# Up projection of two mixture-of-experts layers split into 2x2x2 blocks, seven block products for eight

## The reference

```python
for t in range(S):                       # B, H, S, D = 2, 8, 768, 64
    state = gamma * state + einsum('bhd,bhe->bhde', k[:, :, t], v[:, :, t])
    y[:, :, t] = scale * einsum('bhd,bhde->bhe', q[:, :, t], state)
for e in range(E):                       # N, D, F = 1536, 512, 1024; E = 8, then 4
    h = np.maximum(x @ w1[e], 0.0)       # up projection
    out += P[:, e:e + 1] * (h @ w2[e])   # down projection
```

## Time and profile before

| | |
|---|---|
| median of three runs | 1670.83 us (1670.52 to 1671.59) |
| span of the profiled execution | 1668.0 us |
| TensorE busy | 1658.2 us (99%), 7656 matmul records |
| VectorE, ScalarE, GpSimd busy | 490.5, 296.9, 44.1 us |
| DMA | 64.23 MB, mean 39 GB/s |

### The profile page before, as it was taken

The page is one execution under the profiler, slowest core; times in us unless marked ns, Lnnn a source line. Parts: engine busy times, 40 slices in busy tenths (PEclk is TensorE's granted clock), DMA queues, the critical chain, the costliest instruction groups (busy, mean ns, idle before and its releaser), DMA issues.

```text
span 1668.0 us, 18690 instructions
## 1 busy us (share of the span) xinstructions
PE 1658.2 (99%) x7656; PEld 1374.9 (82%) x7656; DVE 490.5 (29%) x793; ACT 296.9 (18%) x487; POOL 44.1 (3%) x62
## 2 busy tenths in 40 slices
PE   8999999999999999999999999999999999999999
PEld 7988888888888888888888888888888888888887
DVE  5752332332232132132133123225123213213211
ACT  2321221221121121121121122113112112112111
POOL 3310000000000000000000000001000000000000
PEclk9999999999999999999999999999999999999999
DMA  8520110010011011011011011001001101101000
GB/s 177 122 102 1 51 51 0 3 67 32 0 50 50 0 50 50 0 50 50 0 50 50 0 50 51 0 0 66 36 0 51 50 0 50 50 0 50 25 25 25
DMA packets 62157, 64.23 MB, mean 39 GB/s; under 512 B 40240, under 2 KB 42416, under 8 KB 62128
## 3 DMA queue, kind: packets, MB, share of 16 engines
q1 hardware_dynamic: 47248, 58.99, 10.7%
q10 hardware_dynamic: 14880, 4.83, 1.2%
HBM read 60.67 MB, written 3.15 MB: 38 GB/s over the span
## 4 chain that ended last, share of the span: by engine, by line
PE 99%; issue 1%; DVE 0%; POOL 0%; SPq 0%; POOLq 0%; DVEq 0%
PE bank L707 16%; PE bank L705 16%; PE bank L682 16%; PE bank L686 16%; PE bank L684 16%; PE bank L709 16%; PE bank L580 2%; PE bank L607 1%; PE bank L592 1%; PE bank L598 1%; PE bank L569 0%; PE bank L659 0%; PE bank L563 0%; PE bank L642 0%; PE bank L644 0%
## 5 line engine op out<-in xcount | busy, mean ns | idle before, releaser
L707 PE MATMUL bank<-w_lo,h_hi 128*128 128x512 f32 x1152 | 453.7, 394 | 0.0
L705 PE MATMUL bank<-w_hi,h_hi 128*128 128x512 f32 x1152 | 452.3, 393 | 0.0
L682 PE MATMUL bank<-x_hi,w_hi 128*128 128x512 f32 x1152 | 448.5, 389 | 0.0
L684 PE MATMUL bank<-x_lo,w_hi 128*128 128x512 f32 x1152 | 448.2, 389 | 0.0
L686 PE MATMUL bank<-x_hi,w_lo 128*128 128x512 f32 x1152 | 448.1, 389 | 0.0
L709 PE MATMUL bank<-w_hi,h_lo 128*128 128x512 f32 x1152 | 447.2, 388 | 0.0
L358 ACT ACTIVATE h_hi<-bank 128x512 fp32r<-128x512 f32 x288 | 172.2, 598 | 1255.2 <-PE bank L686 1255.2
L505 DVE SCALAR_TENSOR_TENSOR h_lo<-bank,h_hi 128x512 fp32r<-128x512 f32 x288 | 199.2, 692 | 545.1 <-ACT h_hi L358 545.1
L515 DVE SCALAR_TENSOR_TENSOR acc<-bank,gate,acc 128x512 f32<-128x512 f32 x144 | 101.0, 750 | 566.0 <-PE bank L709 566.0
L705 PEld LDWEIGHTS bank<-w_hi,h_hi 128*128 128x128 f32 x1152 | 216.3, 188 | 50.0
L709 PEld LDWEIGHTS bank<-w_hi,h_lo 128*128 128x128 f32 x1152 | 216.2, 188 | 48.4
(11 more groups left out here) (62 smaller groups left out, 251.6 us busy)
## 6 DMA issues: line engine op xcount, KB each, us to landing
w_raw<-in_moe_w SPq DMA_DIRECT2D x23, 2048.0 KB, 8.1
k_in<-in_k SPq DMA_DIRECT2D x12, 256.0 KB, 3.8
q_in<-in_q SPq DMA_DIRECT2D x12, 256.0 KB, 4.5
v_in<-in_v ACTq DMA_DIRECT2D x10, 256.0 KB, 3.0
w_raw<-in_moe_w ACTq DMA_DIRECT2D x4, 512.0 KB, 4.8
out<-acc SPq DMA_DIRECT2D x2, 1024.0 KB, 4.3
out<-acc SPq DMA_DIRECT2D x4, 256.0 KB, 2.1
mask<-in_c_mask SPq DMA_DIRECT2D x1, 512.0 KB, 6.3
```

Of the source, the lines that this page charges most:

```text
L682: nc.tensor.matmul(up_bank[f % 2][:, :], w1_hi[:, c, fs], x_hi[:, c, cols], start=(c == 0), stop=False)
L684: nc.tensor.matmul(up_bank[f % 2][:, :], w1_hi[:, c, fs], x_lo[:, c, cols], start=False, stop=False)
L705: nc.tensor.matmul(down_bank[u][:, :], h_hi[:, f, rows], w2_hi[:, f, :], start=(f == 0), stop=False)
L707: nc.tensor.matmul(down_bank[u][:, :], h_hi[:, f, rows], w2_lo[:, f, :], start=False, stop=False)
```

## The change

Each half expert (512 of the 1024 columns of w1, and the matching rows of w2) is now a unit, 24 in all. Within it the up projection is seen as a 2x2 block matrix times a 2x2 block matrix: features in two halves of 256, hidden columns in two halves of 256, and tokens in two halves, which are the two batches. Instead of eight block products it makes seven, of sums and differences of blocks, and adds their results:

```diff
+PRODUCTS = [
+    (W_A11, X_B11, ON_X, True),
+    (W_S2, X_T2, ON_X, False),
+    (W_S3, X_T3, ON_Y, True),
+    (W_S1, X_T1, ON_X, False),
+    (W_S4, X_B22, ON_X, False),
+    (W_A12, X_B21, ON_Z, True),
+    (W_A22, X_T4, ON_Y, False),
+]
...
-        x_hi = sb("x_hi", [P, DC, NTOK], F32R)
...
-        w1_hi = sb("w1_hi", [P, DC, FF], F32R)
...
+        x_hi = sb("x_hi", [P, 7, 2, SEQ], F32R)
...
+        w1_hi = sb("w1_hi", [P, 7, 2, 2 * P], F32R)
...
+        w1_sum = sb("w1_sum", [P, 3, 2, 2 * P])
...
+            ups = sb("ups", [P, 2, 3, BLK], F32, moe)
```

TensorE goes twice through each unit, with blocks of 384 tokens of each batch (`PAIRS` = 2, `CPB` = 3). X, Y and Z are PSUM bank pairs, one bank for each half of 128 hidden columns:

```diff
+            def up(k, p, first=False, gates_out=False, x2=None):
...
+                for n, (w, x, kind, start) in enumerate(PRODUCTS):
+                    if p == 0:
+                        pe.wait_ge(w1_ready, 4 * k + {W_A11: 1, W_S1: 1, W_S2: 2, W_S3: 2, W_S4: 3}.get(w, 4))
...
+                    for half in range(2):
+                        if first and n == 0 and half == 0:
+                            pe.wait_ge(xlo_ready, 3 * CPB)
+                        if first and n == 5 and half == 0:
+                            pe.wait_ge(y_drained, STEPS)
+                        if n == 1:
+                            pe.wait_ge(copied, copies_before(k, p) + (half + 1))
+                        elif n == 3:
+                            pe.wait_ge(copied, copies_before(k, p) + (2 + half + 1))
+                        elif n == 4:
+                            pe.wait_ge(copied, copies_before(k, p) + (4 + half + 1))
+                        elif n == 6:
+                            pe.wait_ge(summed, sums_before(k, p) + (half + 1))
...
+                        for kc in range(2):
+                            nc.tensor.matmul(o, w1_hi[:, w, kc, fs], x_hi[:, x, kc, at],
+                                             start=start and kc == 0, stop=False, skip_group_check=True)
+                            nc.tensor.matmul(o, w1_hi[:, w, kc, fs], x_lo[:, x, kc, at],
+                                             start=False, stop=False, skip_group_check=True)
+                            last = nc.tensor.matmul(o, w1_lo[:, w, kc, fs], x_hi[:, x, kc, at],
+                                                    start=False, stop=kc == 1, skip_group_check=True)
+                        last.then_inc(up_done, 1)
```

ScalarE copies three partial results of X per half to SBUF (`hidden_copy`, behind products 0, 1 and 3) and still applies ReLU; VectorE adds Y or Z to them (`hidden_sum`, 6 per pass of 384 columns) and makes `h_lo` (8 per pass):

```diff
+            def hidden_copy(k, p, prod, half, slot):
+                act.wait_ge(up_done, ups_before(k, p) + (2 * prod + half + 1))
+                nc.scalar.copy(ups[:, half, slot, :], up_psum(ON_X, half)).then_inc(copied, 1)
...
+            def hidden_sum(k, p, n, half, slot, kind):
+                nc.vector.tensor_tensor(ups[:, half, slot, :], up_psum(kind, half), ups[:, half, slot, :],
+                                        ALU.add).then_inc(summed, 1)
```

VectorE makes the sums of the w1 blocks (`w1_sums`, four of 512 columns) and now also casts w2 (`split_w2`, four operations of 1024 columns). The loads of w1 and w2 are halves of 1 MB each, all from SP's queue. VectorE's order for one unit:

```diff
+            def unit(k, gate, col, how="add"):
+                split_w2(k)
+                hidden(k, 0)
+                down(k, 0, gate, col, how)
+                w1_sums(k + 1)
+                hidden(k, 1)
+                down(k, 1, gate, col, how, split_next=True)
```

The x blocks' sums (`x_sums`, four of 256 columns) and low parts (512, 512 and 768 columns) are GpSimd's, per chunk of 128 tokens of both batches, in the attention and between the layers (there the first two low parts are VectorE's). `y_dec` has three buffers in turn. In the attention the loops are written out; VectorE's queue towards its end:

```diff
+            for s in range(STEPS):
+                c, b = s // BATCH, s % BATCH
+                mask_scores(s)
...
+                y_out(s, b, c)
+                if s == STEPS - 4:
+                    w1_sums(0, first=True)
+                if s == STEPS - 2:
...
+                    split_w1_low(0, 0)
+                    split_w1_low(0, 1)
+            split_w1_low(0, 2)
+            split_w1_low(0, 3)
```

The start of the experts on TensorE and on ScalarE, where `y1_high` makes the high parts of the last five x blocks of a chunk (`logits` waits for all low parts of x, `xlo_ready` 3 * CH; TensorE's lines stand first):

```diff
+            up(0, 0, first=True)
+            logits()
...
+            pe.wait_ge(logits_out, 2)
+            down(0, 0, first=True)
+            gates()
+            up(0, 1, gates_out=True)
...
+            unit(0, 0)
+            y1_high(CH - 1)
+            logits_to_sbuf()
```

More of the change, by code:

```diff
@@ L187, in _ @@
             load_v(0, 1)
-            with sp.Fori(0, CH - 1) as c:
+            for c in range(CH - 1):
                 for b in range(BATCH):
@@ new lines, in scale_acc, with down @@
+            def scale_acc(p):
+                for u in range(2 * CPB):
+                    i = row_of(p, u)
+                    dve.wait_ge(acc_written, downs_before(1, p) + (u + 1))
+                    nc.vector.tensor_scalar(acc[:, i, :], acc[:, i, :], gate1[:, i, 0:1], None,
+                                            ALU.mult).then_inc(acc_scaled, 1)
+            def down(k, p, gate, col, how="add", split_next=False):
+                for u in range(2 * CPB):
+                    add_expert(k, p, u, gate, col, how)
+                    if split_next and u < 4:
+                        split_w1_low(k + 1, u)
@@ L557, in _ @@
+            down(L2_LAST, 1, gate2, E2 - 1)
         @block.tensor
@@ new lines, in down @@
+            def down(k, p, first=False, x2=None):
+                if p == 0:
+                    pe.wait_ge(w2_ready, 2 * k + 2)
+                for u in range(2 * CPB):
+                    b, rows = (1 if u < CPB else 0), slice(u % CPB * P, (u % CPB + 1) * P)
+                    if not (first and u < 2):
+                        pe.wait_ge(acc_written, downs_before(k, p) + (u - 1))
+                    for n, f in enumerate([2, 0, 3, 1] if b else [0, 1, 2, 3]):
+                        if u == 0 or u == CPB:
+                            pe.wait_ge(h_ready, h_before(k, p) + (n + 1 if b else n + 5))
+                        o = down_bank[u % 2][:, :]
+                        nc.tensor.matmul(o, h_hi[:, f, b, rows], w2_hi[:, f, :], start=(n == 0), stop=False)
+                        nc.tensor.matmul(o, h_hi[:, f, b, rows], w2_lo[:, f, :], start=False, stop=False)
+                        last = nc.tensor.matmul(o, h_lo[:, f, b, rows], w2_hi[:, f, :],
+                                                start=False, stop=(n == UC - 1))
+                    last.then_inc(down_done, 1)
+                    if x2 is not None and u == 0:
+                        transpose_x2(x2 + 1)
+                    if x2 is not None and u == CPB:
+                        transpose_x2(x2 + 2)
@@ new lines, in unit @@
+            def unit(k):
+                for p in range(PAIRS):
+                    up(k, p)
+                    down(k, p)
+            up(0, 0, first=True)
[4 more added lines that the diff above has]
+            up(0, 1, gates_out=True)
+            down(0, 1)
+            unit(1)
+            unit(2)
+            unit(3)
+            with pe.Fori(2, E1 - 1) as e:
+                unit(2 * e)
+                unit(2 * e + 1)
@@ L745, in _constants @@
+            down(L1_LAST + 1, 1)
+            unit(L1_LAST + 2)
+            with pe.Fori(E1 + 1, E1 + E2 - 1) as e:
+                unit(2 * e)
+                unit(2 * e + 1)
+            unit(L2_LAST - 1)
+            unit(L2_LAST)
 def _constants():
```

799 lines of the change are left out of this document (490 added, 309 removed).

## The result

The changed kernel takes 1623.71 us (median of 4 runs, 1619.68 to 1624.01) against 1670.67 us for the kernel before on the same chip: a ratio of 0.9711, 95% interval 0.9697 to 0.9725. That is 47.0 us less where 64.1 were forecast, so 17.1 us did not come; the time itself lies 16.7 above the forecast 1607. One run of the kernel of experiment 2 took 2041.54 us at a granted clock of 0.751, a slow state of the chip, and is left out everywhere.

A forecast was written before the change was run, and what follows sets the result against it. TensorE was taken as the bound, busy 1658.2 of 1668.0 us. 84.6 us gained in the up projection less 20.5 given back is 64.1, so 1670.8 - 64.1 = 1607 us; range 1588 to 1640.

The forecast's parts named there:

- the up projection: 4032 matmuls of 384 columns at 173.3 ns replace 3456 of 512: a gain of 84.6 us.
- The down projection: Same 3456 matmuls of 512 columns in another order: 0 us, at most 7 us either way.
- The waits inside a pass: PSUM copies ahead of products 1 and 4 come in time: cost 0, margin 0.06 us for the load.
- Rival 1: Copies out of PSUM come late, 0.1 to 0.3 us in 192 places: costs 19 to 58 us; chance 0.12.
- Rival 2: Weight load binds up matmuls, 193 ns apart or more: 1686 us, slower than before; chance 0.08.
- Rival 3: Narrow matmuls carry hardly any surplus over their 160 ns stream: 1553 us in all; chance 0.04.
- VectorE, ScalarE, the loads: VectorE busy 36 of 62 us per half expert, ScalarE less, w2 split before its sum: cost 0.
- The attention: VectorE's four w1 sums cost 1.0 us, two w1 low parts ahead of the last masks 2.4 us.
- Start of the experts: First up pass: waits of 1.4 us ahead of product 6 and 7.1 us ahead of the logits.
- Clock and layer change: Low clock after the gap ahead of the logits, 3.4 us; x2's route between the layers, twice, 3.6 us.
- The worst case of 1626 us: Total time with 7 us for the down projection and the other bounds at their worst.

The follow-up runs named there:

- experiment 2: Changed kernel with the down projection's sub-tiles taken two at a time, in two banks in turn: 1624.14 us, ratio 0.9720.
- experiment 6: Kernel before, two separate edits: GpSimd's four opening semaphore increments moved to VectorE, 1669.58 us; GpSimd's attention loop written out, 1670.80 us.
- experiment 5: Changed kernel with ScalarE's last two x casts ahead of its ReLUs: 1616.12 us; with 192-byte pad 1597.57; GpSimd also waiting for VectorE's casts 1595.19.

## Why the prediction was right, and where not

**What bounds the kernel, and the up projection: right.** 4032 matmuls at 173.3 ns (173.6 on average) is what happened, and the surplus is a constant 13.3 ns, not a share, which the 256 and 384 columns with w1 as weights show. By the formula of the Trainium skill (TensorE: Matmul & The Clock Gate, Back-to-back issue gap) 384 columns would take 162.5 ns; the trace disagrees at every width tried. The section gives the formula for a matmul by itself and not for a stream of them, which the prediction did not say.

**The down projection: the step that failed.** "Its 228.6 against 226.7 ns show that the operands' placement is worth 2 ns, so it moves by at most 7 us either way." The cause named was the right one and its size was not: two placements had been seen, and their difference was taken for the bound on a third. The distances by placement run from 226.7 to 234 ns, and this change moved h from 229 to 233.3. With what the experiments showed the bounds would have been -7 and +17 us; from the rows before, the upper one could not be had, and the prediction should have called it open, since the tiles' new places were not worked out. The term measured +15.2 over all down matmuls (+16.2 by the pass above).

**The waits inside a pass: right.** No pass waits at product 1 or 4. Rival 1 (late copies) falls by the 7.2 us of idle time of L1001 in all. Rival 2 (the weight load binds) falls by 173.3 ns against a load record of 188, and the narrow groups put the least distance at 111 ns. Rival 3 (hardly any surplus) falls by the 13.3 ns.

**VectorE, ScalarE, the loads: right.** VectorE is busy for 337 of the 628 us from 400 to 1028, ten half experts, so 34 each with 36 forecast, and no product 6 in the loop waited for the split of w2.

**The attention: right in its losses, blind to a gain.** The w1 sums and the two low parts ahead of the last masks cost 3.4 us by the forecast. The product of scores and v of step 8 started at 62.39 before and at 58.13 after, a lead of 4.3 us; the first up matmul had a lead of 1.0 only. So 3.3 us were lost on the way, at the two waits for VectorE's masks in the timeline above (1.22 and 1.44 us, and what follows them). The lead itself was not forecast. By the traces it comes from GpSimd's start, 3.5 us earlier, and from the clock: between 9.1 and 15.9 us it stood at 0.52 before and at 1.00 after. No run tells the two apart, as neither edit of experiment 6 moved that start.

**Start of the experts: right.** 1.7 us ahead of product 6 (1.4) and 7.6 ahead of the logits (7.1), by the steps worked out, each 3 to 4 us earlier than forecast, as the attention ended earlier; experiment 5 removed the second by moving the step that the forecast named.

**Clock and layer change: right in kind, too small.** The forecast gave the low clock to one gap. It followed all three: the one of 7.6 us ahead of the logits, and the two of 3.5 and 2.4 us between the layers, 6.7 us against 3.4. The layer change itself took 5.9 against 3.6. The small terms behind the attention came out 6.1 us too low in all, the attention 4.4 too high; 1.7 us of error are left of them beside the 16.2 of the down projection. That they nearly cancel is luck. The worst case of 1626 us does not come out of the stated bounds either: 7, 1.7, 3.1 and 4.4 us above 1606.7 make 1623.

## What to carry to other kernels

A term of "nothing changes here" needs the same look as the others when tiles move in SBUF: here it was worth 15 us of 64, and a pad of 192 bytes won it back, and 7.6 us in the old kernel as well. When matmuls bound a kernel, take the distance of their starts tile by tile, not the mean length of a record, and ask of two that differ what differs in their weights. And price the edges of a phase as gap plus slow clock: in these runs gaps of 2.6 to 7.7 us between starts, amid long stretches of matmuls, went with 3.4 to 10.2 us of low clock, some of it within the gap. The amount varied from run to run, and one gap of 2.6 us brought none.

## What was not expected of the hardware

- The start of a 128x128 float32r weight tile within 256 bytes of its partition sets the distance of 512-column matmuls: 226.7 ns at 128, 229 at 64, 232.2 to 233.5 at 0, 233.1 to 234 at 32, 160, 192 and 224. At 384 columns, 192 against 128, it is about 1 ns. Why is not shown.
- The surplus of a float32r matmul over its stream is 13.3 ns at 256, 384 and 512 columns with the weights at 128 modulo 256, and at 192 and 128 columns matmuls that each load their weights start about 111 ns apart.
- VectorE's cast of two 1024-column tiles took 1.30 us alone and 3.8 us beside GpSimd's subtractions; a subtraction of GpSimd took 2.18 in place of 1.29 us beside VectorE's.
